# A fused linear-attention, gated-MLP and channel-mix kernel: where r is scaled, and how the halves of three weights are made

## The reference, cut to what matters

```python
# attention: 2 batches x 8 heads, 768 steps, head size 48
for t in range(S):
    y[:, :, t] = r_t @ (state + (u * k_t) v_t^T)
    state = w_t[..., None] * state + k_t v_t^T
x = y as [2, 768, 384]                       # heads side by side
# gated MLP
h = gelu_tanh(x @ w_in); u, v = halves of h  # w_in 384 x 1024
v_n = layernorm(v) * g_ln
v_s = einsum('ts,bsd->btd', w_sg, v_n) + b_sg # w_sg 768 x 768, the gate weight
x = x + (u * v_s) @ w_out                    # w_out 512 x 384
# channel mix
xk, xr = mixes of x and x shifted by one step
out = sigmoid(xr @ w_r) * (relu(xk @ w_k)**2 @ w_v)
```

## Time and profile before

| | us |
|---|---|
| median of 3 runs | 423.65 (422.62 to 425.02) |
| the profiled execution | 422.52, of which its span is 420.8 |
| PE busy | 368.8 (88% of the span) |
| DVE busy | 260.1 (62%) |
| ACT busy | 182.2 (43%) |
| POOL busy | 125.0 (30%) |

### The profile page before, as it was taken

The page is one execution under the profiler, slowest core; times in us unless marked ns, Lnnn a source line. Parts: engine busy times, 40 slices in busy tenths (PEclk is TensorE's granted clock), DMA queues, the critical chain, the costliest instruction groups (busy, mean ns, idle before and its releaser), DMA issues.

```text
span 420.8 us, 9110 instructions
## 1 busy us (share of the span) xinstructions
PE 368.8 (88%) x3836; PEld 347.9 (83%) x3836; DVE 260.1 (62%) x380; ACT 182.2 (43%) x312; POOL 125.0 (30%) x141
## 2 busy tenths in 40 slices
PE   4656758879697899949999999999999999999997
PEld 3445647667596787849998999999999999999996
DVE  6467889797979983571645535998796311764011
ACT  3644627364554544543312406626783800565100
POOL 5936535271625732100000000520970000473000
PEclk9887869698888999959999999999999999999999
DMA  7997281716202101100100000305000011000011
GB/s 133 195 259 156 48 202 47 162 50 113 58 4 58 31 3 30 30 2 20 47 2 0 0 2 4 147 0 176 33 2 0 2 37 58 19 2 0 19 39 56
DMA packets 58840, 23.59 MB, mean 56 GB/s; under 512 B 52912, under 2 KB 56368, under 8 KB 58800
## 3 DMA queue, kind: packets, MB, share of 16 engines
q1 hardware_dynamic: 58800, 23.02, 22.1%
HBM read 18.29 MB, written 2.36 MB: 49 GB/s over the span
## 4 chain that ended last, share of the span: by engine, by line
PE 78%; issue 8%; ACT 6%; DVE 5%; SPq 1%; DMA 1%; POOL 0%; DVEq 0%; ACTq 0%; POOLq 0%
PE ps L1201 20%; PE ps L1202 19%; PE ps L1203 19%; PE ps L1192 4%; PE ps L1124 4%; PE ps L1188 3%; PE ps L1146 3%; PE ps L1134 2%; DVE kT L863 1%; PE ps L1157 1%; ACT ktok L651 1%; DVE sc L908 1%; PE ps L1129 1%; ACT rU L630 1%; ACT r L633 1%
## 5 line engine op out<-in xcount | busy, mean ns | idle before, releaser
L565 POOL TENSOR_TENSOR r<-r,wb 112x768 f32<-112x768 f32 x24 | 42.2, 1762 | 83.1 <-PE ps L1192 82.4
L613 POOL TENSOR_TENSOR sq_f<-sq_f 128x384 f32<-128x384 f32 x32 | 33.8, 1071 | 74.9 <-ACT sq_f L753 74.8
L863 DVE TENSOR_TENSOR kT<-kT,wb 112x384 f32<-112x384 f32 x40 | 37.9, 949 | 19.0 <-PE ps L1192 18.9
L1192 PE MATMUL ps<-r,kT 112*64 112x64 f32 x960 | 38.9, 238 | 7.1 <-DVE kT L863 4.3
L1192 PEld LDWEIGHTS ps<-r,kT 112*64 112x64 f32 x960 | 34.5, 150 | 12.7 <-issue 6.8
L1039 DVE TENSOR_TENSOR ot<-ps,ee 128x384 f32<-128x384 f32 x12 | 6.7, 558 | 54.6 <-PE ps L1203 54.6
L1024 DVE TENSOR_TENSOR sq_l<-sq_f,sq_h 128x384 fp32r<-128x384 f32 x32 | 27.7, 864 | 10.4 <-ACT sq_h L758 10.4
L1203 PE MATMUL ps<-xk_h,wk_l 128*128 128x384 f32 x96 | 32.2, 335 | 0.0
L1202 PE MATMUL ps<-xk_l,wk_h 128*128 128x384 f32 x96 | 32.2, 335 | 0.0
L1201 PE MATMUL ps<-xk_h,wk_h 128*128 128x384 f32 x96 | 32.2, 335 | 0.0
L1201 PE MATMUL ps<-wv_h,sq_h 128*128 128x384 f32 x96 | 32.1, 334 | 0.0
(11 more groups left out here) (146 smaller groups left out, 971.2 us busy)
## 6 DMA issues: line engine op xcount, KB each, us to landing
tok_w<-in_w_dram SPq DMA_DIRECT2D x16, 144.0 KB, 3.2
tok_k<-in_k_dram SPq DMA_DIRECT2D x16, 144.0 KB, 3.2
tok_r<-in_r_dram SPq DMA_DIRECT2D x16, 144.0 KB, 3.2
sgn<-in_moe_w_sg_dram SPq DMA_DIRECT2D x6, 384.0 KB, 3.9
vt<-in_v_dram SPq DMA_DIRECT2D x32, 72.0 KB, 2.6
out_dram<-ot SPq DMA_DIRECT2D x12, 192.0 KB, 1.9
xT<-yT SPq DMA_DIRECT2D x12, 144.0 KB, 2.6
win_raw<-in_moe_w_in_dram SPq DMA_DIRECT2D x1, 1536.0 KB, 7.5
```

The source lines that it names most:

```text
L565: nc.gpsimd.tensor_tensor(t, t, pair_of(h, 0, q).unsqueeze(1).unsqueeze(3).broadcast_to([ROWS, 2, S // (2 * h), h]), ALU.mult).then_inc(r_ ...
L613: nc.gpsimd.tensor_tensor(t, t, t, ALU.mult).then_inc(k_sq, 1)
L863: nc.vector.tensor_tensor(t, t, pair_of(h, 1, q).unsqueeze(2).broadcast_to([ROWS, S // (2 * h), h]), ALU.mult).then_inc(k_scaled, 1)
L1192: ins = nc.tensor.matmul(level_bank(l)[CHUNK[g], c * CH:(c + 1) * CH].rearrange("p (x t) -> p x t", x=2), kT[q % 4][0:ROWS, s], right2(r2[ ...
```

## The change

Four things. First, DVE does `first_r` of an odd slot at the place of PE's r job, which is behind level 5 of the oldest pair and ahead of levels 3 and 1, instead of behind all levels. (`first_k` keeps its place: in an even slot PE's k job follows the last level anyway.) Second, the gate weight's turn is copied by ACT as plain float32 into `wsg_f`, which lies on the memory of `wsg_l`; `low_sg` and PE's wait for it are gone. Its high halves are six new ACT casts (128x768 each) at the end of slots 15 (1), 16 (2), 17 (2) and 18 (1), its low halves six new DVE subtractions, from SBUF, at the end of slots' level work in 16 (1), 17 (2), 18 (2) and 19 (1), ahead of the layer norm (18) and its application (19). Third, the high pieces of w_in are made in slots 2, 2, 3, 4, 4, 5 instead of 2 to 7, and their low pieces at the head of slots 3, 3, 4, 5, 5, 6 instead of the end of slots 3 to 8. Fourth, the high pieces of w_out go from slots 15 to 17 to slots 20, 20, 21, their low ones to slot 21.

```diff
-        R_SCALES += [(q, l) for q, l in level_jobs(slot) if 0 < l < DVE_R]
         R_SCALES += [(q, 0) for kind, q, *_ in side_jobs(slot) if kind == "r"]
+        R_SCALES += [(q, l) for q, l in level_jobs(slot) if 0 < l < DVE_R]
...
+    HIGH_SLOTS = {("in", 0): 2, ("in", 1): 2, ("in", 2): 3, ("in", 3): 4, ("in", 4): 4, ("in", 5): 5,
+                  ("sg", 0): 15, ("sg", 1): 16, ("sg", 2): 16, ("sg", 3): 17, ("sg", 4): 17, ("sg", 5): 18,
+                  ("out", 0): 20, ("out", 1): 20, ("out", 2): 21}
+    LOW_SLOTS = {("in", 0): 3, ("in", 1): 3, ("in", 2): 4, ("in", 3): 5, ("in", 4): 5, ("in", 5): 6,
+                 ("sg", 0): 16, ("sg", 1): 17, ("sg", 2): 17, ("sg", 3): 18, ("sg", 4): 18, ("sg", 5): 19,
+                 ("out", 0): 21, ("out", 1): 21, ("out", 2): 21}
...
+        wsg_f = at("wsg_f", [P, C, S], F32, A_sg + SG)
...
-                    nc.scalar.copy(wsg_h[:, :, q * P:(q + 1) * P].rearrange("p (b j) t -> p b j t", b=2),
+                    nc.scalar.copy(wsg_f[:, :, q * P:(q + 1) * P].rearrange("p (b j) t -> p b j t", b=2),
                                    src[:, :, 0:HF].rearrange("p b (j t) -> p b j t", j=3)).then_inc(copied, 1)
...
+            def high_half(piece):
+                kind, n = piece
+                _, raw, hi = halves(piece)
+                if kind == "sg":
+                    act.wait_ge(copied, turn_at[("sg", C - 1)] + 1)
+                else:
+                    act.wait_ge(win_in if kind == "in" else wout_in, 16)
+                nc.scalar.copy(hi, raw).then_inc(w_high, 1)
...
-                if slot in SPLITS:
...
+                for piece in PIECE_LIST:
+                    if HIGH_SLOTS[piece] == slot:
+                        high_half(piece)
...
-            def low_sg(n):
...
             for slot in range(SLOTS):
+                for n, piece in enumerate(PIECE_LIST):
+                    if LOW_SLOTS[piece] == slot and slot < 2 * LEVELS:
+                        low_half(n)
                 for job in pe_jobs(slot):
                     if job[0] == "level":
...
-                    elif job[0] == "sg":
-                        low_sg(job[1])
-                for job in side_jobs(slot):
-                    if job[0] == "k":
-                        first_k(job[1])
                     elif job[0] == "r":
                         first_r(job[1])
-                    elif job[0] == "u":
+                    elif job[0] == "k":
+                        first_k(job[1])
+                for job in side_jobs(slot):
+                    if job[0] == "u":
                         chain(job[1])
...
-                for n in range(PIECES):
-                    if LOW_SLOTS[n] == slot:
+                for n, piece in enumerate(PIECE_LIST):
+                    if LOW_SLOTS[piece] == slot and slot >= 2 * LEVELS:
                         low_half(n)
...
-                elif last[0] == "sg":
-                    pe.wait_ge(sg_low, last[1] + 1)
...
-                        pe.wait_ge(sg_low, C)
+                        pe.wait_ge(w_low, split_at("sg"))
```

More of the change, by code:

```diff
@@ L93, in rwkv_gmlp_channel_mix_kernel @@
         K_SCALES += [(q, l) for q, l in level_jobs(slot) if l] + [(q, 0) for kind, q, *_ in side_jobs(slot) if kind == "k"]
+        R_SCALES += [(q, 0) for kind, q, *_ in side_jobs(slot) if kind == "r"]
         R_SCALES += [(q, l) for q, l in level_jobs(slot) if 0 < l < DVE_R]
-        R_SCALES += [(q, 0) for kind, q, *_ in side_jobs(slot) if kind == "r"]
     POOL_SCALES = [(q, l) for q, l in LEVEL_JOBS if l >= DVE_R]
@@ L115, in join_at @@
         return JOINS.index((q, l)) + 1
[L117 to L120, removed]
+    HIGH_SLOTS = {("in", 0): 2, ("in", 1): 2, ("in", 2): 3, ("in", 3): 4, ("in", 4): 4, ("in", 5): 5,
[4 more added lines that the diff above has]
+                 ("out", 0): 21, ("out", 1): 21, ("out", 2): 21}
+    PIECE_LIST = list(HIGH_SLOTS)
+    PIECES = len(PIECE_LIST)
     def split_at(kind):
-        return max(n + 1 for n, piece in enumerate(SPLITS.values()) if piece[0] == kind)
+        return max(n + 1 for n, piece in enumerate(PIECE_LIST) if piece[0] == kind)
     def segments(q):
@@ L316, in rwkv_gmlp_channel_mix_kernel @@
         r_odd_out = sem("r_odd_out")
-        sg_low = sem("sg_low")
         k_scaled = sem("k_scaled")
@@ L403, in halves @@
                 return win_l[:, m, c], win_raw[:, m, c], win_h[:, m, c]
+            if kind == "sg":
+                return wsg_l[:, n, :], wsg_f[:, n, :], wsg_h[:, n, :]
             return [t.ap().rearrange("p f d -> p (f d)")[:, n * FH:(n + 1) * FH] for t in (wout_l, wout_raw, wout_h)]
@@ L916, in low_half @@
             def low_half(n):
-                lo, raw, hi = halves(list(SPLITS.values())[n])
+                lo, raw, hi = halves(PIECE_LIST[n])
                 dve.wait_ge(w_high, n + 1)
                 nc.vector.tensor_tensor(lo, raw, hi.bitcast(F32), ALU.subtract).then_inc(w_low, 1)
-            def low_sg(n):
[L923 to L928, removed]
             def low_x(b, m):
```

## The result

| | before | changed |
|---|---|---|
| median, us | 424.33 (4 runs, 422.62 to 425.53) | 402.82 (4 runs, 400.42 to 404.04) |
| profiled execution, us (span) | 422.52 (420.8) | 404.04 (402.3) |

What follows compares the result with a forecast made beforehand. PE's w turn waiting for `first_r` on DVE, then level 2, was taken to set a pair's 19 us. Terms: -1.9 - 2.3 - 3 x 3.3 - 1.0 + 2.1 = -13.0 us on 422.52, 409.5; median 410.6, range 404 to 419.

Steps and rivals of the forecast that it cites:

- clock term: Per pair, w turn, level 2, sg and level 0 on PE may keep 2.4 GHz: 0.6 us, ends 0 and 1.4.
- `first_r` moved: Per pair, `first_r` ahead of levels 3 and 1 on DVE starts level 2 earlier: 2.5 us, ends 2.1 and 2.9.
- `low_sg`: Its removal from slots 4 to 14, between levels 2 and 0 on DVE: 0.2 us per pair, ends 0 and 0.5.
- Three pairs: The pairs with a w turn behind a scan: 3.3 us gain each, ends 2.1 and 4.8.
- Slots 12 to 14: The 15.73 us scan-to-scan period without a w turn: 1.0 us gain, ends 0 and 1.8.
- Up to the first scan: Slots 1 to 6: 1.9 us gain up to level 2 at 39.61, then 2.3 to the first scan.
- The w_in places: Removing w_in's low half behind a scan only moves DVE's wait for POOL: nothing credited.
- Late slots: Gate weight's new casts and subtractions in slots 15 to 19: +2.1 us, ends 0 and 8.8.
- Rival B: PE's clock stays full: three pairs gain 4.5 us each, -18.2 us in all, 405.4; chance 0.22.
- C: DVE reaches level 1's `scale_r` just behind a POOL product again, a new wait: -4.5 us, 419.1; chance 0.20.
- D: Late casts and subtractions in slots 15 to 19 outweigh the gains: +4 us, 427.8; chance 0.08.
- The forecast's middle between the clocks: Per pair, 0.6 us taken for PE's clock between ends 0 and 1.4; the forecast's chance was 0.46.

Runs made afterwards that it cites:

- filler_before: The kernel before with 14 or 20 unread identity transposes issued by PE where it idles before the w turn (slots 4, 6 to 12): 417.28 us, ratio 0.9835.
- twice_ahead: The changed kernel with the two products of `first_r` made twice in slots 1 to 13, first into unused memory: 402.17 us, ratio 0.9516.
- firstr_sg: The changed kernel with the w_in pieces back at the ends of slots 2 to 7 (high) and 3 to 8 (low): 402.52 us, ratio 0.9499.
- no_firstr: The changed kernel with `first_r` back behind all levels: 423.86 us, ratio 0.9981 to the kernel before.
- best: Changed kernel, last ktok copy earlier, gate weight's halves in slots 7 to 17 (three low ones behind `first_r`), filler transposes in three ktok waits: 399.00 us, ratio 0.9401.

## Why the prediction was wrong

The mechanism was right: w waited for `first_r`, the move frees it, level 2 waits for `scale_r` instead, and the half clock goes. The sizes of the terms of a pair were not: 3.3 us forecast, 5.1 measured. The step that failed first is the clock term.

- The clock: 0.6 us per pair, upper end 1.4. In slot 12 level 2, sg and level 0 gave back 1.81 (0.56 + 0.66 + 0.59), and filler_before, which changes nothing else, gives 1.87 with the w turn's share. I had called sg and level 0 together "about the same again" as level 2's 0.63, but each is. And I took less than half of the end for safety without a row that spoke for a half clock remaining. The 0.7 us of idle time before level 2 did not keep it down.
- `first_r` moved: 2.5 us for level 2's start, ends 2.1 and 2.9; measured 3.3 (11.90 to 8.60). I had let the waiting hide 0.8 us of the 1.28 put in ahead; the waiting hid all of it, because `scale_r` still arrives just behind POOL's product and ends where that lets it. twice_ahead shows that even twice as much leaves the stretch as long. The waiting to read was that in all three of DVE's scales, not in one.
- `low_sg`: 0.2 us, upper end 0.5; 1.22 behind the other two. I priced it in the slack of the kernel before. Once PE comes earlier, the same instruction is on the path: a price taken from the old path does not hold for the second edit.
- The two rows of a pair that add up are 3.30 us for level 2's start and 1.82 behind it, 5.12. The 1.22 of `low_sg` is no further gain on top: it is what would have been lost of the 1.82 had it stayed.
- Three pairs: -9.9 forecast, -15.3 measured, outside the ends of the terms taken together (14.4). Slots 12 to 14: -1.0, and -2.6.
- Up to the first scan: -4.2 forecast, -4.3 measured. The closeness is luck: six other profiles with the same code up to there give -4.38 to -2.25, and the 3.68 us wait of slot 6 is in none of the terms.
- The w_in places: nothing forecast, nothing in the total (firstr_sg), by a loss in slots 5 and 6 and a gain behind them.
- Late slots: +2.1 forecast, 0.7 of waits measured in no_firstr; the norm came 0.8 us later, not 1.4, and most of that fell into ACT's idle time. With the clock of that one execution it was +3.6.

One reading of the prediction was too wide: of the seven waits of 15.0 us before line 1124, the turns of w are five, 14.0 us.

Rival B came nearest, by the pairs at full clock: its -18.2 us stands beside -18.5 in the profiles. That is luck in part, since three pairs and slots 12 to 14 gained 2.6 us more than it had, and the start and the late slots 2.2 less. Its 405.4 is still 2.6 above the median. C and D did not happen: DVE did come just behind POOL, but not later than before. B's chance of 0.22 was too low. The forecast's middle between the clocks is not what the changed kernel did: its four stretches from 61.47 to 116.11 us were all at 1.00. Other versions do have such a stretch in between (firstr_sg's first, 16.00 us at 0.89).

## What to carry to other kernels

Free work on a waiting engine is found by what the wait is for. If an engine loses its time to another engine's product and not to its own queue, work that does not compete with that product can be put ahead, up to the length of the waiting (here 1.13 us of it in front of a wait of 1.33 in `scale_r`); what it delays on the way has to have slack as well. When one edit takes a wait away, reprice the others on the new path before adding up; here two edits worth 3.5% and 0% were worth 5.1% together. And idle time of PE is worth more than its length where the clock falls behind it; filler matmuls in the gap measure that share alone.

## What the runs showed of the hardware that was not expected

- Transposes that nobody reads, 2.35 us of them in a gap of 3.3 us, kept PE's granted clock at 1.00 (2.4 GHz) through three stretches that had 0.82 to 0.91, and made the kernel 1.65% faster (0.9785 to 0.9884), 1.3 to 2.0 us per pair.
- A start 0.10 to 0.19 us earlier or later decides 1.3 us: `scale_r` took 0.95 us when DVE was ahead of POOL and 2.28 when it was 0.14 us behind, and POOL's product 2.15 to 2.24 instead of 1.60.
- Two subtractions or products of equal length on DVE differ in what they do to POOL: with an input in PSUM nothing (POOL's join took 1.00 us in twice_ahead, at 92.63 beside `first_r`), with both in SBUF 0.7 us (1.71 in best).
